# Attention and two MLP layers on one core: key moves split around two loads, one score group a slot sooner, weight low parts spread over four slots

## What is computed

```python
def _attn_ref(q, k, v, alpha):            # each (4, 8, 768, 48)
    state = np.zeros((B, H, D, D), dtype=np.float32)
    for t in range(S):
        state = alpha[:, :, t, :, None] * state + np.einsum('bhd,bhe->bhde', k[:, :, t], v[:, :, t])
        y[:, :, t] = np.einsum('bhd,bhde->bhe', q[:, :, t], state)
    return y.astype(np.float32)
def _moe_ref(x, w_in, w_out):             # (3072, 384) x (384, 2048) x (2048, 384)
    h = x @ w_in
    return ((h - np.tanh(h)) @ w_out).astype(np.float32)
def _moe2_ref(x, w_in, w_out, alpha):
    h = x @ w_in
    g = np.maximum(h, 0.0) + alpha * np.minimum(h, 0.0)
    return (g @ w_out).astype(np.float32)
```

## Time and profile before

| | us |
|---|---|
| median of 3 runs | 933.98 |
| lowest and highest | 931.97, 934.57 |
| the profiled execution | 936.59 |
| its span | 934.9 |
| PE busy | 907.0 (97%) |
| DVE busy | 565.8 (61%) |
| ACT busy | 326.8 (35%) |
| POOL busy | 208.6 (22%) |
| mean granted clock of TensorE | 0.985 |

### The profile page before, as it was taken

How to read it: one execution, slowest core, us unless ns; L and a number is a source line. 1 busy time by engine, 2 the same in 40 slices (tenths; PEclk the granted TensorE clock), 3 DMA queues, 4 the chain that set the end, 5 groups by cost and what they waited for, 6 DMA issues and landing times.

```text
span 934.9 us, 22771 instructions
## 1 busy us (share of the span) xinstructions
PE 907.0 (97%) x9918; PEld 748.7 (80%) x9918; DVE 565.8 (61%) x713; ACT 326.8 (35%) x534; POOL 208.6 (22%) x193
## 2 busy tenths in 40 slices
PE   3799999999999999999999999999999999999998
PEld 3678888888888788878888888888888888888886
DVE  7898848656764776377444455465555655554553
ACT  6753633354344425332544531211211211212212
POOL 7734504332350434043314420000000000000000
PEclk8699999999999999999999999999999999999999
DMA  8560072036005403610053010010100200100000
GB/s 285 149 225 2 6 220 74 3 76 220 3 3 144 152 2 59 201 38 3 2 197 142 1 68 1 1 67 0 66 2 0 67 0 0 67 0 0 34 1 34
DMA packets 24965, 61.05 MB, mean 65 GB/s; under 512 B 3216, under 2 KB 11408, under 8 KB 22352
## 3 DMA queue, kind: packets, MB, share of 16 engines
q1 hardware_dynamic: 24880, 59.79, 20.5%
HBM read 46.15 MB, written 9.44 MB: 59 GB/s over the span
## 4 chain that ended last, share of the span: by engine, by line
PE 95%; POOL 1%; issue 1%; DVE 1%; DMA 1%; ACT 0%; POOLq 0%; DVEq 0%
PE ph L727 42%; PE acc L736 15%; PE acc L738 14%; PE acc L737 14%; PE ps L540 4%; PE ps L613 1%; PE py L613 1%; POOL k_t L1261 1%; DVE w_lo L1157 1%; PE py L609 1%; PE ps L609 1%; PE ps L527 1%; PE ps L534 1%; DMA q_early<-q 1%; PE py L678 0%
## 5 line engine op out<-in xcount | busy, mean ns | idle before, releaser
L936 ACT ACTIVATE g_hi<-g 128x512 fp32r<-128x512 f32 x192 | 121.2, 631 | 425.1 <-PE acc L738 338.5
L1182 DVE TENSOR_TENSOR g_lo<-g,g_hi 128x512 fp32r<-128x512 f32 x192 | 145.1, 756 | 187.4 <-ACT g_hi L936 186.6
L736 PE MATMUL acc<-g_lo,w_hi 128*128 128x512 f32 x576 | 227.1, 394 | 3.1 <-issue 1.9
L737 PE MATMUL acc<-g_hi,w_lo 128*128 128x512 f32 x576 | 224.6, 390 | 0.0
L738 PE MATMUL acc<-g_hi,w_hi 128*128 128x512 f32 x576 | 224.5, 390 | 0.0
L727 PE MATMUL ph<-x_hi,w_lo 128*128 128x512 f32 x576 | 166.0, 397 | 0.0
L727 PE MATMUL ph<-x_hi,w_hi 128*128 128x512 f32 x576 | 162.6, 391 | 0.0
L727 PE MATMUL ph<-x_lo,w_hi 128*128 128x512 f32 x576 | 162.0, 389 | 0.0
L736 PEld LDWEIGHTS acc<-g_lo,w_hi 128*128 128x128 f32 x576 | 108.1, 188 | 25.9 <-DVE g_lo L1182 3.1
L737 PEld LDWEIGHTS acc<-g_hi,w_lo 128*128 128x128 f32 x576 | 108.2, 188 | 24.0 <-issue 2.1
L727 PEld LDWEIGHTS ph<-x_hi,w_hi 128*128 128x128 f32 x576 | 108.5, 188 | 23.2
(11 more groups left out here) (140 smaller groups left out, 618.0 us busy)
## 6 DMA issues: line engine op xcount, KB each, us to landing
v_t<-v SPq DMA_DIRECT2D x6, 1024.0 KB, 8.0
a_t<-alpha SPq DMA_DIRECT2D x5, 1024.0 KB, 5.3
k_t<-k SPq DMA_DIRECT2D x5, 1024.0 KB, 7.1
x<-x_out SPq DMA_DIRECT2D x6, 768.0 KB, 9.6
x_in<-x SPq DMA_DIRECT2D x6, 768.0 KB, 4.9
kT<-trees SPq DMA_DIRECT2D x64, 64.0 KB, 2.0
q_w<-q SPq DMA_DIRECT2D x10, 384.0 KB, 5.7
out<-prob SPq DMA_DIRECT2D x5, 768.0 KB, 3.8
```

The lines of the kernel that those rows point to most:

```text
L736: pe.matmul(acc[:, m, :], w_hi[:, f, part], g_lo[:, f % 2, :], start=(f == 0), stop=False)
L737: pe.matmul(acc[:, m, :], w_lo[:, f, part], g_hi[:, f % 2, :], start=False, stop=False)
L936: act.activation(g_hi[:, f % 2, :], g[:, f % 2, :], ACT.Copy).then_inc(g_hi_made, 1)
L1182: dve.tensor_tensor(g_lo[:, f % 2, :], g[:, f % 2, :], g_hi[:, f % 2, :].bitcast(F32), ALU.subtract).then_inc(g_lo_made, 1)
```

## The change

Three edits. `load_tile` issues half of the 16 moves, then alpha and k, then the other half. For tile 5 group 1 stands behind slot 2 (in 2) instead of slot 3 (out 0). The low parts of weights 3, 7, 8, 9 and 10, made in slots 0, 0, 0, 1 and 2, are made in slots 0, 1, 2, 2 and 3.

```diff
-           4: (3, 7, 12, 15, 18, 20, 22), 5: (3, 7, 12, 15, 17, 20, 22)}
+           4: (3, 7, 12, 15, 18, 20, 22), 5: (2, 7, 12, 15, 17, 20, 22)}
...
-W_LO_BESIDE = {0: [3, 7, 8], 1: [9], 2: [10], 9: [11], 11: [12], 18: [13], 23: [14], 24: [15]}
+W_LO_BESIDE = {0: [3], 1: [7], 2: [8, 9], 3: [10], 9: [11], 11: [12], 18: [13], 23: [14], 24: [15]}
...
-            def move_k_turned():
+            def move_k_turned(tokens):
...
+            def load_a_and_k(a):
+                sp.wait_ge(y_done, B * a)
+                sp.dma_start(a_t[:, :], alpha[bass.ds(a * 128, 128), :]).then_inc(ld_a[LANES], 16)
+                if is_tile(a, 1):
+                    sp.wait_ge(kT_done, B)
+                sp.dma_start(k_t[:, :], k[bass.ds(a * 128, 128), :]).then_inc(ld_k[LANES], 16)
...
                 if not is_tile(a, 1):
                     sp.wait_ge(turned, B * n)
                     sp.wait_ge(st_done, LANES * n)
-                    move_k_turned()
-                sp.wait_ge(y_done, B * a)
-                sp.dma_start(a_t[:, :], alpha[bass.ds(a * 128, 128), :]).then_inc(ld_a[LANES], 16)
-                if is_tile(a, 1):
-                    sp.wait_ge(kT_done, B)
-                sp.dma_start(k_t[:, :], k[bass.ds(a * 128, 128), :]).then_inc(ld_k[LANES], 16)
+                    for tokens in range(NB // 2):
+                        move_k_turned(tokens)
+                load_a_and_k(a)
+                if not is_tile(a, 1):
+                    for tokens in range(NB // 2, NB):
+                        move_k_turned(tokens)
```

More of the change, by code:

```diff
@@ L412, in load_v @@
                 sp.dma_start(v_t[:, :], v[bass.ds(a * C, C), :]).then_inc(ld_v, 16)
-            def move_k_turned():
[L416 to L419, removed]
+            def move_k_turned(tokens):
+                for features in range(4):
+                    sp.dma_start(kT[32 * tokens:32 * tokens + 32, features, :],
+                                 k_turned[32 * features:32 * features + 32, tokens, :]).then_inc(ld_kT, 16)
+            def load_a_and_k(a):
[4 more added lines that the diff above has]
+                sp.dma_start(k_t[:, :], k[bass.ds(a * 128, 128), :]).then_inc(ld_k[LANES], 16)
             def load_tile(a):
```

## The result

| | before | changed |
|---|---|---|
| median, us | 933.74 (6 runs) | 938.38 (6 runs) |
| lowest and highest | 931.97, 934.57 | 937.94, 941.73 |
| profiled execution | 936.59 | 937.94 |
| its span | 934.9 | 936.2 |

The ratio is 1.0058, with a 95% interval of 1.0047 to 1.0069: 4.6 us more. I had forecast 934.8 and "the same". The profiled execution of the changed kernel is only 1.4 us over that of before: the one of before lies 2.9 us above its median and held the pause of the last stage (3.65 us by my estimate with the half clock), the one of the changed kernel is the lowest of its six.

A forecast was written before the change was run, and what follows sets the result against it. The prediction took TensorE (PE), busy 97% of the span, as the bound. Terms +0.85 + 0 + 0 put the median from 933.98 to 934.8 us, with an 8 in 10 range of 931.7 to 938.0.

The forecast's parts named there:

- the pause of the last stage: Last stage, PE idle 1.95 us between two matmuls, then half clock: 3.65 us together; rival that it goes: 931.2, chance 0.08.
- Part 2: Alpha and k issued between two eights of moves, four stages: moves still land before PE needs them, cost 0.
- PE's demand: State product in the stages of tiles 2 to 5: PE due at about 390.1, 10.9 us behind alpha's issue.
- The term behind it: Second eight moves, after k lands at 386.9: 0.26 us each, 2.1 for eight, so the last lands at 389.0.
- The 7.1: Load of k in the four stages: k lands 7.1 us after its issue, at 386.9.
- The slack of 1.1: State product: the last move lands at 389.0, 1.1 us before PE needs it, so PE does not wait.
- that rival: Moves land late and PE waits at the state product in four stages; at 1 us each 938.8; chance 0.14.
- Part 1: Low parts of weights spread, stage from 45 us: 1.15 us gained before out 0, given back at in 7 and out 5; +0.85 us.
- 1.15 us surely: PE's wait before out 0 for g_lo(0), stage from 45 us: the gain the change could surely touch, 1.15 us.
- The half clock that I allowed for: Rival: the two new waits near 76 and 79 us halve the clock for a while, +1.7 us, 936.5; chance 0.10.
- Part 3: Group 1 of the last tile a slot sooner, last stage: cost 0, slack 0.8 us.

The follow-up runs named there:

- part 2 alone: Only alpha and k issued between the two eights of moves, slots and low parts as before, against the kernel before: 937.62 us against 933.22, ratio 1.0047.

## Why the prediction was wrong

**Part 2 is where it failed, in one term: when the last move lands.** "the second eight queue behind 2 MB. k lands 7.1 after its issue: 386.9" and "0.26 us each, 2.1 for eight: 389.0". Issuing was no part of it: the last move's issue ended 6.2 us behind the start of alpha's, where I had counted 7.2. PE's demand was right (11.1 us behind alpha's issue against 10.9). The step that failed is k's landing. It came 9.6 us behind its issue in that stage (8.3 to 10.1 over the four), not 7.1, and the last move 12.4 behind alpha's issue, not 9.8. Of these 2.6 us, 2.5 are k's. The term behind it held: the last move landed 2.2 us behind k, against 2.1. That is in part luck, since the first moves went beside k's last packets and then took longer than 0.26 us each. The 7.1 was read where no move stood behind k, and I used it for a k with eight behind it. The slack of 1.1 became waits of 1.0, 0.7, 0.5 and 1.3 us.

The price of that rival was right in size: "At 1 us each 4 us, 938.8", measured 938.38 with 3.4 us of waits. The clock did not fall behind any of the four waits (granted clock 1.00 in the 3 to 4 us behind each). What was wrong is its chance, 0.14: with a slack of 1.1 us at the end of a sum of 9.8, an error of 11% was enough. I also said "Decides from 1.1 us more than I count"; the count was off by 2.6.

**Part 1 was right** in its places: no wait at out 0, new ones "near 76 (for g(5)) and 79 (for g_lo(5))", seen at 76.93 and 79.46. Sizes: 0.6 and 0.2 us instead of 1.3 and 0.7. VectorE stood better than I had it at g_lo(4), which ran 67.82 to 68.5, ahead of POOL, and not behind it; the pair ended at 73.45, not 74.2. Against the earlier trace rows out 5 starts 0.1 us later, in a stage that began some 0.45 us sooner: + 0.6 against my + 0.85. The half clock that I allowed for did not come.

What was wrong in it is "1.15 us surely". The old wait hangs on a race of two instructions, and kernels with the same low parts do not always lose it. In the earlier trace rows POOL's product began 0.13 us ahead of g_lo(0), which then took 2.38 us. With the same low parts and alpha alone between the moves, g_lo(0) was ahead and took 0.68, and PE had no wait:

```profile
52.70 0.68 DVE L1189 TENSOR_TENSOR g_lo<-g,g_hi 128x512 fp32r<-128x512 f32 x1
52.91 2.23 POOL L1247 TENSOR_TENSOR a_t<-a_t 128x1024 f32<-128x1024 f32 x1 [4.53 <-DMA a_t<-alpha]
```

Of the seven kernels with the old low parts, one profiled execution each, five have the wait (1.0 to 1.3 us) and two have not, though these seven differ only in what is done some 60 us later and on; of the five with low parts moved none has it. So what taking it away gains in the median can be less than 1.15 us, and a part of the 1.2 us by which alpha alone between the moves lay under before may be this; how large a part is not shown.

**Part 3 was right** at nothing. The pause behind it, which I held for a possible gain of 3.65, has other lengths in other executions; nothing here ties it to the edit.

**The sum.** + 0.6 from part 1 and + 3.4 from part 2 make 4.0 of the 4.6; part 2 alone measured + 4.4 with an interval of 2.9 to 6.0. The rest is within that.

## What to carry to other kernels

When a small transfer that the bounding engine needs soon is put behind large ones that it doesn't need yet, don't use a landing time that was read without them: with eight 64 KB moves queued behind it, the k load took 8.3 to 10.1 us instead of 7.1, and the last move landed 11.2 to 12.4 us behind the first load's issue. Ask who waits for each transfer first; here nobody on TensorE waited for alpha or k, so the reordering had nothing to gain there and some 3.4 us of slack to lose, in every stage.

Work moved on an engine that is busy 8.28 of 8.5 us is not hidden; look for the slot behind its last deadline (here behind g_lo(5)), not for the next slot. And before a wait of 1 us is counted as a sure gain, look by how much it was lost: here two instructions started 0.13 us apart.

## What the runs showed of the hardware

- Loads issued on another engine's queue did not get out of the way of the moves: k took 11.6 us, against 8.9 on the shared queue with eight moves behind it and 7.1 with none.
- On one queue the packets of the moves came behind those of k but for the last ones, and yet k moved at 292 GB/s with eight moves behind it and at 414 with none.
- The order of small SBUF-to-SBUF moves mattered where they piled up: with four in a row on different groups of 32 partitions the last one landed 0.7 us sooner out of 11.8, with nothing else changed in the program.
- VectorE's products of two SBUF tensors and POOL's products took turns by whole instructions, and who came first decided: the same pair of q products took 3.68 us with VectorE first and 5.02 with POOL first, where each of the two took some 2.5 instead of 1.23.
